# Two linear layers of Strassen-like products behind an attention: weight operands read back from memory, q's subtraction and scaling on GpSimd, one x sum in a place of its own

## What is computed

```python
q_s = softmax_over_head_dim(q)            # exp(q - max) / (sum + 1e-9), 8 batches, 8 heads, 576 rows, 64
k_s = softmax_over_rows(k)
x = q_s @ (k_s.T @ v)                     # per batch and head; gathered as 4608 tokens x 512
g = x @ w_gate;  val = x @ w_val          # 512 -> 1536
x = (g * sigmoid(g) * val) @ w_out        # 1536 -> 512          (layer 1)
h = max(x @ w1, x @ w2, x @ w3)           # 512 -> 768
out = h @ w_out2                          # 768 -> 512           (layer 2)
```

## Time and profile before

| | |
|---|---|
| median of three runs (lowest, highest) | 1741.77 us (1736.96, 1746.33) |
| the profiled execution | 1751.78 us |
| its span, first to last instruction | 1750.0 us |
| mean granted TensorE clock | 0.95 of full |
| busy: PE, DVE, ACT, POOL | 1558.6, 940.8, 718.5, 1225.4 us |
| DMA packets moved | 163.92 MB |
| a load of a group's weights, issue to landing (median) | 3.7 us for 512 KB |
| a load of a quarter of x, the four of them issued together | 6.4 us for 512 KB |

### The profile page before, as it was taken

One profiled execution on the slowest core, in us unless ns is written; L12 is line 12 of the kernel. 1 busy time (PEld: TensorE's weight loads), 2 busy tenths in 40 slices (PEclk: granted clock), 3 DMA queues, 4 the chain that ended last, 5 costly groups with the idle time before them and its releaser, 6 DMA issues.

```text
span 1750.0 us, 21089 instructions
## 1 busy us (share of the span) xinstructions
PE 1558.6 (89%) x7002; PEld 1271.3 (73%) x7002; DVE 940.8 (54%) x1437; ACT 718.5 (41%) x1308; POOL 1225.4 (70%) x1030
## 2 busy tenths in 40 slices
PE   8688879989799997999988998799899899799898
PEld 7566757777677775777766777688678678678787
DVE  6655278684776845566453444533543543443433
ACT  4433255443454544444353333434334343343443
POOL 5322396656965669756697657977887887887897
PEclk9888989999999999999998999899999999999999
DMA  8434423333143431421212112132132122122131
GB/s 231 136 118 122 149 87 117 109 115 109 59 145 109 135 116 46 127 67 62 98 49 96 49 37 96 37 108 87 36 105 87 49 97 84 61 91 79 60 121 61
DMA packets 101804, 163.92 MB, mean 94 GB/s; under 512 B 8000, under 2 KB 54080, under 8 KB 101696
## 3 DMA queue, kind: packets, MB, share of 16 engines
q1 hardware_dynamic: 96512, 153.12, 27.7%
q10 hardware_dynamic: 5184, 9.44, 1.7%
HBM read 134.22 MB, written 28.31 MB: 93 GB/s over the span
## 4 chain that ended last, share of the span: by engine, by line
PE 55%; POOL 25%; DVE 9%; issue 6%; ACT 4%; DMA 1%; SPq 0%; ACTq 0%; DVEq 0%; POOLq 0%
PE round L1381 8%; PE round L1383 7%; PE round L1384 7%; PE y_bank L1406 6%; PE y_bank L1408 6%; PE y_bank L1407 5%; POOL h L516 5%; POOL wring L500 5%; POOL wout L510 4%; PE third_bank L1381 3%; PE third_bank L1384 3%; PE third_bank L1383 3%; POOL xops L532 2%; PE att_bank L1319 2%; POOL combos L479 1%
## 5 line engine op out<-in xcount | busy, mean ns | idle before, releaser
L1381 PE MATMUL round<-xops,wring 128*128 128x512 f32 (+1 forms) x930 | 367.9, 396 | 53.4 <-DVE c L1116 17.3
L1383 PE MATMUL round<-xops,wring 128*128 128x512 f32 (+1 forms) x930 | 360.1, 387 | 0.0
L1384 PE MATMUL round<-xops,wring 128*128 128x512 f32 (+1 forms) x930 | 359.3, 386 | 0.0
L1181 DVE TENSOR_TENSOR y_sb<-y_sb,y_bank 128x512 f32<-128x512 f32 x232 | 159.1, 686 | 362.5 <-PE y_bank L1408 361.8
L500 POOL TENSOR_TENSOR wring<-combos,wring 128x512 fp32r<-128x512 f32 x186 | 253.6, 1375 | 120.6 <-ACT wring L903 120.6
L1381 PEld LDWEIGHTS round<-xops,wring 128*128 128x128 f32 x930 | 180.6, 194 | 99.3 <-DVE c L1116 22.0
L516 POOL TENSOR_TENSOR h<-hid,h 128x512 fp32r<-128x512 f32 (+1 forms) x156 | 211.2, 1358 | 34.6 <-ACT h L890 34.5
L1406 PE MATMUL y_bank<-h,wout 128*128 128x512 f32 x384 | 160.3, 418 | 66.1 <-POOL wout L510 66.0
L495 POOL TENSOR_TENSOR wring<-raw,wring 128x512 fp32r<-128x512 f32 x93 | 122.7, 1319 | 123.7 <-ACT wring L900 123.6
L1384 PEld LDWEIGHTS round<-xops,wring 128*128 128x128 f32 x930 | 179.7, 193 | 35.4
L1383 PEld LDWEIGHTS round<-xops,wring 128*128 128x128 f32 x930 | 180.7, 194 | 32.5
(11 more groups left out here) (150 smaller groups left out, 3127.6 us busy)
## 6 DMA issues: line engine op xcount, KB each, us to landing
raw<-w_g SPq DMA_DIRECT2D x93, 512.0 KB, 3.7
wraw<-w_o SPq DMA_DIRECT2D x39, 512.0 KB, 4.4
stage<-x_dram SPq DMA_DIRECT2D x32, 512.0 KB, 6.4
x_dram<-stage SPq DMA_DIRECT2D x16, 576.0 KB, 3.6
x_dram<-y_sb SPq DMA_DIRECT2D x36, 256.0 KB, 2.0
out<-y_sb SPq DMA_DIRECT2D x36, 256.0 KB, 2.1
q_sb<-q SPq DMA_DIRECT2D x45, 192.0 KB, 3.4
kt_sb<-k_t SPq DMA_DIRECT2D x30, 288.0 KB, 3.0
```

The source lines that it names most:

```text
L1181: dve.tensor_tensor(to, to, src, ALU.add).then_inc(y_taken, 1)
L1381: pe.matmul(dst[:, 0:g.cols], hi, x1, start=(i in (1, 5) and c == 0), stop=False, skip_group_check=True)
L1383: pe.matmul(dst[:, 0:g.cols], hi, x2, start=False, stop=False, skip_group_check=True)
L1384: mm = pe.matmul(dst[:, 0:g.cols], lo, x1, start=False, stop=(c == 1), skip_group_check=True)
```

## The change

Weights are made once per layer. The first pair of each layer (groups "made", 21 of 93) makes its operands as before, and SP then stores them in memory (`keep_weights`, `keep_wout`). For the other 72 groups SP loads hi and lo of all seven slots from there straight into `wring`, in four pieces, each as soon as the products of its slots in the group two before are done, and PE waits for these transfers alone; for the other 36 steps SP loads w_out's hi and lo from memory. Layer 1's uncombined quarters are the same numbers as the 36 units of the first block; they are stored from there (`keep_unit`), so pair 0 makes only the combinations, and loads three of its seven slots. q's subtraction and scaling go from DVE to POOL for all batches. S4 is made by POOL as a fourth sum in `sum_x`, in a place that is free (`wraw` in layer 1, `k_sb` in layer 2), and no longer waits for the operand before it. The order changes in three places: the y products of a pair's last step are spread further over the next pair's first step and those before the last step later (PLACES_FIRST, PLACES_LAST), from pair 3 on x is loaded and summed six to seven groups before the pair's end, and in pairs 0 to 2 it is summed at product 1 of the last group but one instead of at product 6.

In the diff, the first new branch of `load_weights` that is shown is that for groups that are not made; the lines on `max_q` and `sum_q` are POOL's, and the same two operations are taken out of DVE's program; the last two pieces are PE's.

```diff
+MADE = [n for n, g in enumerate(GROUPS) if g.pair in (0, PAIRS1)]
+PIECES = ((1, 5), (2, 6), (3, 7), (4,))
...
+PLACES_FIRST = [(0, 5), (0, 2), (0, 6), (0, 3), (0, 7), (1, 1), (1, 5)]
+PLACES_LAST = {1: [(0, 6), (0, 3), (0, 7), (1, 5), (1, 2), (1, 3), (1, 7)],
+               2: [(0, 6), (0, 7), (1, 5), (1, 3), (2, 5), (2, 3), (2, 7)]}
...
-            timed.append((where["product", final - 2, 6] + 0.3, ("load_x", pair + 1)))
-            timed.append((where["product", final - 1, 6] + 0.3, ("sum_x", pair + 1)))
+            if pair < 3:
+                timed.append((where["product", final - 2, 6] + 0.3, ("load_x", pair + 1)))
+                timed.append((where["product", final - 1, 1] + 0.3, ("sum_x", pair + 1)))
+            else:
+                timed.append((where["product", final - 7, 1] + 0.3, ("load_x", pair + 1)))
+                timed.append((where["product", final - 6, 1] + 0.3, ("sum_x", pair + 1)))
...
+            def keep_weights(n):
+                sp.wait_ge(w_lo, lo_before(n + 1))
+                number = source(n)[1]
+                if GROUPS[n].layer == 1:
+                    sp.dma_start(kept1[number, :, 3:, :, :], wring[:, n % 2, 3:, :, :].bitcast(F32)).then_inc(w_kept[n % 2], 16)
+                else:
+                    sp.dma_start(kept2[number], wring[:, n % 2, :, :, :].bitcast(F32)).then_inc(w_kept[n % 2], 16)
...
+            def load_weights(n, piece):
...
+                    sp.wait_ge(done[PIECES[piece][-1]], n - 1)
...
+                    slots = slice(first, last + 1, max(last - first, 1))
+                    sp.dma_start(wring[:, n % 2, slots, :, :].bitcast(F32), kept[number, :, slots, :, :])\
+                      .then_inc(w_in[n % 2][piece], 16)
...
+            def keep_unit(n):
+                j, part = divmod(n, 3)
+                tile = unit_weights(n)
+                sp.wait_ge(unit_lo, n + 1)
...
                 pool.tensor_tensor(part[4], part[0], part[4], ALU.subtract).then_inc(x_summed, 1)
+                pool.wait_ge(x_summed, 4 * pair + 2)
+                pool.tensor_tensor(s4(pair), part[2], part[3], ALU.subtract).then_inc(x_summed, 1)
...
+                elif e[0] == "max_q":
+                    subtract_q(e[1], e[2])
+                elif e[0] == "sum_q":
+                    scale_q(e[1], e[2])
...
-                if i in (1, 5, 6, 3):
-                    pe.wait_ge(w_lo, 4 * n + {1: 1, 5: 2, 6: 3, 3: 4}[i])
+                if made(n) and g.layer == 2:
+                    if i in (1, 5, 6, 3):
+                        pe.wait_ge(w_lo, lo_before(n) + {1: 1, 5: 2, 6: 3, 3: 4}[i])
+                elif made(n) and i in (5, 6):
+                    pe.wait_ge(w_lo, lo_before(n) + {5: 1, 6: 2}[i])
+                elif i < 4 or (i == 4 and not made(n)):
+                    pe.wait_ge(w_in[n % 2][i - 1], 16 * transfers(n, i - 1))
...
-                pe.wait_ge(wout_lo, 2 * s + 2)
+                if wout_made(s):
+                    pe.wait_ge(wout_lo, 2 * wout_number(s) + 2)
+                else:
+                    pe.wait_ge(wout_in[s % 2], 16 * wout_transfers(s))
```

More of the change, by code:

```diff
@@ L131, in closer, with made, made_before, lo_before @@
     return GROUPS[n].kind == (1 if GROUPS[n].layer == 1 else 2)
+MADE = [n for n, g in enumerate(GROUPS) if g.pair in (0, PAIRS1)]
+PIECES = ((1, 5), (2, 6), (3, 7), (4,))
+def made(n):
+    return GROUPS[n].pair in (0, PAIRS1)
+def made_before(n, parity=None):
+    return sum(m < n and parity in (None, m % 2) for m in MADE)
+def lo_before(n):
+    return sum(2 if GROUPS[m].layer == 1 else 4 for m in MADE if m < n)
+def hi_before(n):
+    return sum(1 if GROUPS[m].layer == 1 else 3 for m in MADE if m < n)
+def source(n):
+    g = GROUPS[n]
+    number = n - min(m for m in range(NGROUPS) if GROUPS[m].pair == g.pair)
+    return (0 if g.layer == 1 else min(m for m in MADE if GROUPS[m].layer == 2)) + number, number
 def group_of(step, kind):
@@ L188, in whole_order @@
         ys = [("y", s - 1, k) for k in range(STEPS[s - 1].units)] if s else []
-        places = PLACES_8[step.layer] if len(ys) == 8 else PLACES_4
+        places = places_of(step, len(ys))
         kinds = 2 if step.layer == 1 else 3
@@ L432, in taken, with transfers, wout_made, wout_number @@
             return (c12_ready if t == 1 else c22_ready), n + 1
+        def transfers(n, piece):
+            return sum(1 for m in range(n % 2, n + 1, 2)
+                       if not made(m) or (GROUPS[m].layer == 1 and piece < 3))
+        def wout_made(s):
+            return STEPS[s].pair == PAIRS1
+        def wout_number(s):
+            return sum(wout_made(t) for t in range(s))
+        def wout_transfers(s):
+            return sum(not wout_made(t) for t in range(s % 2, s + 1, 2))
         def units_done(s):
@@ L701, in at_once @@
                 elif e[0] == "product":
                     _, n, i = e
-                    if i == 2 and n + 2 < NGROUPS:
-                        load_weights(n + 2)
-                    if i == 7 and GROUPS[n].kind == 0 and GROUPS[n].step:
-                        load_wout(GROUPS[n].step)
-            def next_after(e):
-                if e[0] == "second" and e[1] == F1 - 1:
-                    for m in range(4):
-                        store_first(m)
+                    after = n + 2
@@ new lines, in next_after @@
+                    if after < NGROUPS:
+                        if made(after):
+                            if i == 2:
+                                load_raw(after)
+                            if GROUPS[after].layer == 1 and i in (1, 2, 3):
+                                load_weights(after, i - 1)
+                        elif made(n):
+                            if i == 4:
+                                for piece in range(len(PIECES)):
+                                    load_weights(after, piece)
+                        elif i in (5, 6, 7, 4):
+                            load_weights(after, (5, 6, 7, 4).index(i))
@@ L712, in next_after @@
+                    if i == 3 and made(n):
+                        keep_weights(n)
+                    s = GROUPS[n].step
+                    if i == 2 and GROUPS[n].kind == 0 and s:
+                        load_wout(s)
+                    if i == 4 and GROUPS[n].kind == 1 and wout_made(s):
+                        keep_wout(s)
                 elif e[0] == "y" and STEPS[e[1]].final:
@@ L741, in _ @@
             store_x(0, 1)
+            for n in range(6):
+                keep_unit(n)
             for n, e in enumerate(order):
```

277 lines of the change are left out of this document (177 added, 100 removed).

## The result

The median of four runs is 1584.8 us (1581.8 to 1587.0), against 1741.0 for the kernel before beside it: ratio 0.910, 95% interval 0.907 to 0.913. The profiled execution took 1585.3 us (span 1583.5).

What follows compares the result with a forecast made beforehand. PE was thought held by late POOL work, chiefly y products waiting for w_out's lo part (66 us), and losses where pairs meet. Terms sum to 127 us off 1751.8, so 1625, less 10 for the median: 1615 us, range 1580 to 1668.

Steps and rivals of the forecast that it cites:

- Only POOL's own waits go: Rival, 20%: DVE and ACT still hold PE at pair seams and beside attention; 80 us won, 1662 us.
- Better everywhere: Rival, 4%: the losses left, 41 us in all, halve and the first block wins 15: 1585 us.
- the losses left: Loss expected to remain: 10, 8, 4, 4, 4, 3 and 8 us in pairs 1, 2, 3, 5, 6, 7 and 8.
- attention stalls stay: Pairs 1 and 2: attention stalls remain, no single row for them; 10 and 8 us left, 16 and 19 won.
- next late: Pair 3: after w_out, lo of h would be late next, 3.4 us and hand-overs, but hidden.
- DVE's 14 us of work in a group of 13: Where pairs meet, DVE has about 14 us of work per group; cited for the rival of 1662 us.
- Pair 3: Once-a-step y wait goes; of a loss of 35 us, 4 left for the pair's start, 31 won.
- the five units: Pair 3: five units (6.8 us) before the first y product hide lo of h's 3.4 us and hand-overs.
- The bounds: q on POOL, first block: between a gain of 15 us and a loss of 10, taken as 6 won.
- q on POOL costs: Rival, 12%: ACT's exponential waits for POOL and two-input work slows both engines; 25 us less won, 1640 us.
- The stores were costed at nothing: Stores of kept operands: cost nothing, up to 10 us of loss in the first block.
- the serial rival: Rival, 4%: each 512 KB piece takes its 3.7 us by itself, so transfers bind: 1781 us.

Runs made afterwards that it cites:

- experiment 6: Kernel before with only w_out's operands stored and loaded from memory, POOL still making all operands of the products: 1670.6 us, ratio 0.957.
- experiment 4: Kernel after, with POOL making unneeded scratch subtractions wherever weight operands are no longer made (busy 1171 us): 1628.0 us, ratio 0.933 to before.
- experiment 5: Kernel after with POOL's scratch work, plus ACT's copies on scratch and the old waits between the two: 1667.3 us, ratio 0.955 to before.
- experiment 2: Kernel after with the old places of y products and old times of x loads and sums: 1582.4 us, ratio 0.907 to before.
- experiment 1: Kernel after with q's subtraction and scaling of batches 1 to 7 back on DVE: 1596.6 us, ratio 0.915 to before.
- experiment 9: Kernel before with only q's subtraction and scaling of batches 1 to 7 moved to POOL: 1729.1 us, ratio 0.992.
- experiment 11: Kernel after with pair 5's x sums at pair 4's end and the first six kept units stored after the first k loads: 1574.0 us, ratio 0.902.
- experiment 3: Kernel after with the load and sums of x for pair 5 at the end of pair 4: 1581.5 us, ratio 0.906 to before.
- 12: Kernel after with old y places and x times, and the first six kept units stored after the first k loads: 1576.2 us, ratio 0.904.
- experiment 7: Kernel after with one 1.8 MB transfer per group, asked for after product 4, instead of four pieces: 1633.0 us, ratio 0.935 to before.
- 10: Kernel before with only the new places of y products and new times of x loads and sums: 1738.1 us, ratio 0.996.

## Why the prediction was right, and where its sizes were off

**The bound and the cause: right.** The y products' wait for w_out's lo part was the largest single loss, and it is shown alone: experiment 6 takes 73 us of work off POOL, all of it w_out's, and wins 70 to 75. The rival "Only POOL's own waits go" was priced at 1662; the kernel of experiment 6 is near to it, with part of the waits left, and gives 1671. Giving work back to the kernel after returns 43 us for POOL's load as such (experiment 4, a lower bound) and 39 more with ACT's copies and the waits between the two (experiment 5). The remaining 74 us of the 156 should be PE's direct waits for its operands, as against the 70 to 75 that experiment 6 wins from the other side for w_out; that is a subtraction, and no run shows it alone.

**The measured time is that of the case given 4%.** "Better everywhere" was priced at 1585, which is what was measured. It had the losses left (41 us) halved and the first block winning 15. The profiles show that some 36 of the 41 went and that the way to pair 0 won 3.5. So that rival's number came true by luck, and the losses left were the term that was wrong.

**What was "left" at the seams: too much.** The terms sum to 39.5 us less than the profiles show; 10 of that the forecast had taken off for the median, which leaves its 30. Pairs 1 and 2 (10 and 8 left) account for 19 of the 39.5, pairs 5 to 7 (4, 4 and 3 left) for 11, pair 8 (8 left) for 2. The step that failed is "attention stalls stay": it was given 10 and 8 us without a row. In pair 1 PE waited 6.3 us for attention before and 4.0 after, so there they mostly stayed but were small. In pair 2 there was no such wait to stay: its 19.3 us idle were 17.7 for w_out and 1.6 for DVE:

```profile
PE y_bank L1406 <- POOL wout L510: 17.7, 6, 7.4
PE round L1381 <- DVE c L1116: 1.6, 1, 1.6
```

The loss that experiment 4 puts back into pair 2 (5.1 us) is not attention either, but y products waiting for the lo part of h (4.4 us in PE's waits there), which is what the prediction named as next late. In pair 1 POOL's load does reach attention: PE's waits there are 12.8 us in experiment 4, with q on POOL behind the scratch work.

At the seams of layer 2 the losses of pair 5 (9.7 us idle before, in four waits) went whole. The 5.95 of the earlier trace rows was one wait of the kind, and DVE's 14 us of work in a group of 13 did not bind: with the same work there pair 5 is at its floor, and in experiment 2, with the old and more crowded seam, it is too. What share of this is POOL's load, and what ACT's waits for POOL, is open, since experiment 5 makes its loss elsewhere in the pair. A small part is the floor: pair 2 takes 192.1 us, below the 194.2 worked out, so a batch's attention costs 12.6 us rather than 14.7.

**Pair 3: right in kind, 4 too little.** It has no entry loss: 179.5 is the floor. lo of h is hidden, as the five units said.

**q: within its bounds, larger, and in another stage too.** The bounds were a gain of 15 and a loss of 10, the value taken 6; experiment 1 measures 9 to 12, experiment 9 on the kernel before 12 against 1741.0 and 18 against the 1747.3 beside it. I put it in the first block. There it shows when the block is timed from its first matmul with w_out to pair 0: 158.4 to 160.3 us in the three kernels with before's block and 147.6 in experiment 9; 155.4 in experiment 1 and 151.3 to 153.3 in the kernel after and the others with q on POOL. In the kernel after it shows also in pair 0 (5 us, though the same pair 0 takes 214.5 to 217.4 us in three traces) and pair 1. The rival "q on POOL costs" has fallen, though POOL's operation is no shorter than DVE's was (1.05 us against 0.98).

**The stores were costed at nothing and were not free.** The way to pair 0 won 3.5 us; with q alone it won 12 to 18 (experiment 9). The first six stores are a part of the difference. The medians say 7.5 us for them (experiment 11 against 3) and 6.2 (12 against 2); in each couple the two intervals overlap slightly, and both point the same way. The traces agree: the first matmul with w_out is at 66.4 to 69.8 us in the eight kernels with these stores in their first place and at 64.0 and 63.7 us in the two that have them later, and pair 0 starts at 218.9 to 222.5 us and at 217.3 and 216.5. The k tile of the wait above was 5.15 us late, where I had weighed the loads behind `keep_unit` as up to 3 us late against a lead of many events. The rest of the block is not faster with the late stores (153.3 and 152.8 us) and 5 us slower than in experiment 9; whether that is the 30 other units' stores, no run shows. The bound of 10 holds, the value of nothing does not.

**The transfers: right.** No wait for them; and the serial rival at 1781 has fallen, since even one late transfer per group, with stalls, gives 1633, and double the traffic 1612. The lead in pair 8 is thin, as said: a transfer of 7.4 us that is asked for at the group's end is up to 3.5 us late there (experiment 7). The anatomy section of the Trainium skill from which the prediction took 2 us per DMA describes DMAs that GpSimd issues; here SP issues them.

**Pair 4: the sum right, its parts not.** The stall of "up to 6" is 9.7 and the stage still won 6.3, so the rest of it won more than was put. The old time of the sums gives back 4 us of it in experiment 3 and 7 in experiment 11.

**S4 and the order** cost or win nothing as a whole that these runs can tell, but the sums in mid-pair are a stall wherever POOL is loaded (pair 4, experiments 5 and 10); no run isolates S4.

## What to carry to other kernels

When an engine is short, three kernels help to size what it costs: give its load back on scratch, give its neighbour's work and waits for it back as well, and take only the directly awaited work away. Read in the traces where each loss falls before setting it equal to the old one: a pair can be as long as before for another reason. A loss that is left standing in a sum needs a row, just as one that is won does. And where operands are kept in memory for later use, refill in pieces as each slot falls free, and keep a store that waits for its producer behind the loads that others need in the same queue.

## What the runs showed of the hardware

A DVE operation with two operands in SBUF and an operation of POOL's took longer where they met than apart. In experiment 4 one of the x operands' second parts on DVE and a scratch subtraction on POOL meet:

```profile
869.74 1.23 DVE L1391 TENSOR_TENSOR xops<-stage,xops 128x1024 fp32r<-128x1024 f32 x1 [1.91 <-ACT xops L1147]
869.85 2.02 POOL L566 TENSOR_TENSOR scratch<-scratch 128x512 f32<-128x512 f32 x1
```

The scratch subtraction before that one, at 867.62, takes 1.04 us. Here POOL's takes 1 us longer, and DVE's, which began first, 1.23 us where the mean is 1.67. In experiment 6 it is DVE's that gets longer: the same operation takes 2.82 us at 877.62, inside POOL's part of x (2.85 us from 876.51; the median of such a part is 2.41 in the kernel after) and the lo part behind it. The Trainium skill, SBUF — State Buffer, Who interferes with whom, has DVE and GpSimd share one pair of ports, held by one at a time; both places agree.

How busy POOL is does not decide it. The means of these DVE operations in the kernel after, in experiment 4 (POOL busy 1171 us) and in experiment 2 (659):

```profile
L1368 DVE TENSOR_TENSOR xops<-stage,xops 128x1024 fp32r<-128x1024 f32 x24 | 41.3, 1721 | 23.1 <-ACT xops L1124 22.9
...
L1391 DVE TENSOR_TENSOR xops<-stage,xops 128x1024 fp32r<-128x1024 f32 x24 | 40.0, 1665 | 23.5 <-ACT xops L1147 23.4
...
L1362 DVE TENSOR_TENSOR xops<-stage,xops 128x1024 fp32r<-128x1024 f32 x24 | 52.6, 2193 | 9.4 <-ACT xops L1118 8.5
```

They took 2054 ns before. POOL's load alone does not lengthen them, and the old order does. It moves POOL's sums of x to the pair's end, next to these operations; that it is the sums they meet is my reading, not tested. Sums with an operand in PSUM kept their time (698 ns against 696). With the shorter `hid<-hid,c` operations this makes some 20 us of the difference between DVE's 812 us and the 840 that I forecast. I had weighed the rule as speaking against q on POOL; q's gain on either kernel goes the other way.

The DMA queue moved 357 GB/s for a whole pair at a share of 0.97, with copies from memory to memory among it, more than the 341 of the earlier trace rows.
